# Attention with top-32, an MLP and routed experts on one core: top-k over folded scores, mask on ScalarE and GpSimd, exponential and turn moved back

## The chip, the cores and the metric

One core of a Trainium2 chip runs the whole program. The metric is the device time of one execution in microseconds (us); less is better. The engines are PE (TensorE; PEld its weight loads), DVE (VectorE), ACT (ScalarE), POOL (GpSimd) and SP (SyncE, which issues the loads).

## The reference, cut to what matters

Four batches of eight heads, 576 tokens, 64 wide:

```python
scores = scale * np.matmul(q, k.transpose(0, 1, 3, 2))          # 576 x 576 for each head
kth = np.partition(scores, -32, axis=-1)[..., -32:-31]
scores = np.where(scores >= kth, scores, -1000000000.0)
attn = np.exp(scores - np.max(scores, axis=-1, keepdims=True))
attn = attn / (np.sum(attn, axis=-1, keepdims=True) + 1e-09)
x = np.matmul(attn, v)                                         # then 2304 x 512
h = x @ w_in                                                   # 512 x 2048
g = np.where(h > 0.0, h, np.exp(np.minimum(h, 0.0)) - 1.0)
x = g @ w_out                                                  # 2048 x 512
# then one of eight experts (512 x 1024 x 512) for each token, by cosine similarity with expert_emb
```

## The kernel before, in words

**Tiles and slots.** A pair of heads takes nine tiles of 128 queries by 576 keys: four groups of two tiles (one for each head), and a fifth group with one mixed tile that holds the last 64 queries of both heads. There are 16 pairs, so 144 tiles. All engines run a loop over slots `s`, written out in Python, one tile entering in each; what an engine does in slot `s`, and in which order, is the order of the calls in its loop. Waits are on semaphores, and each engine works in order.

**One tile through the engines (before).** PE makes the scores in halves of 288 keys (`score`, L479 and L486) in two PSUM banks, ACT copies them to SBUF (`score_evac`, L682). DVE finds the 32 largest of each row: `eight` (L844) is a MAX8 over 576 columns, `without` (L848) a MATCH_REPLACE over 576 columns that strikes those eight out; four of the one and three of the other for a tile, the second half of one tile's chain interleaved with the first half of the next one's. `bias` (L853) gives the row maximum to ACT, which takes the exponential at once (`expo`, L688). DVE's `mask` (L859) compares the scores with the 32nd largest, multiplies the exponential with that and sums the row. PE turns the masked tile (`turn`, L494, five transposes; with the last tile of a group a sixth one, L498, turns the reciprocals that POOL spread out in `widen`, L355), two slots after the tile entered. ACT copies the turned tile (`turned`, L698), PE multiplies it with the values (`weigh`, L515), DVE multiplies with the reciprocals (`normalise`, L884).

**The MLP beside it.** `mlp_schedule` gives 71 positions for a batch, two to a slot: 32 chunks of the hidden layer (L534, 12 matmuls in fp32r: high and low parts), 32 sums of the second layer (L543, eight instructions each, some split finer so that there are 36 positions), and the row tiles (L552, L559), which go to DRAM. The MLP of batch `b` runs in the slots of batch `b + 1`, beginning `LAG` = 6 slots into it; so it starts in slot 42. For batches 0 to 2 it is beside attention; that of batch 3 is alone. A hidden chunk goes PE, ACT (L728 `Relu(-x)` to `elu_e`, L729 `Relu(x)` to `g`, which frees the PSUM bank, L732 `Exp`), POOL (L396, L398: minus one, add). Only in batch 3 DVE does POOL's part in one instruction (L933).

**After that** come the routing (DVE, PE) and a loop over the experts' tiles on PE (L643, L653).

The order of PE's loop in a slot: `prep` (turning the next pair's q and k, in slots 3 to 5 of a pair), `score(G, 0)` or nothing, `mlp` position 0, `turn(s - 2)`, `score(G, 1)`, `mlp` position 1, `weigh`. On DVE a wait in a chain is this:

```python
def settled(self, but=0):
    if self.n > but:
        dve.wait_ge(dve_step, self.n - but)
```

Of the kernel before, what the change touches and what calls it, by code (L numbers as in the profile page):

```python
# [5 lines left out]
ALU = mybir.AluOpType  # L6
# [7 lines left out]
P = 128  # L14
TOP_K = 32
NEG = -3.0e38


def attention_moe_program(nc, q, k, v, w_in, w_out, emb, tau, w1, w2, out):
# [26 lines left out]
    LAG = 6  # L46
# [5 lines left out]
    with ctx:  # L52
# [9 lines left out]
        ones = sbuf(ctx, "ones", [R, R])  # L62
# [3 lines left out]
        top = sbuf(ctx, "top", [P, 2, TOP_K])  # L66
        negmax = sbuf(ctx, "negmax", [P, 2])
        rowsum = sbuf(ctx, "rowsum", [P, 2, 2])
        rowrec = sbuf(ctx, "rowrec", [P, 2, 2])
        rec_b = sbuf(ctx, "rec_b", [P, 2, P])  # L70
# [17 lines left out]
        q_t = sbuf(first, "q_t", [P, 2, FULL * P])  # L88
# [4 lines left out]
        work = sbuf(first, "work", [P, 2, S])  # L93
        probs_t = sbuf(first, "probs_t", [P, 3, (NCH + 1) * P])
        x_f = sbuf(first, "x_f", [P, S])
        probs = sbuf(first, "probs", [P, 2, NCH * P])
        x2_t = sbuf(first, "x2_t", [P, KD, HS])
        elu_e = sbuf(first, "elu_e", [P, HS])
# [33 lines left out]
        def bank(name):  # L132
# [15 lines left out]
        rowmax, exp_done, mask_done, rec_done = (  # L148
            sem("rowmax"), sem("exp_done"), sem("mask_done"), sem("rec_done"))
        rec_wide = sem("rec_wide")  # L150
# [4 lines left out]
        elu_neg, elu_exp, elu_less = sem("elu_neg"), sem("elu_exp"), sem("elu_less")  # L155
# [53 lines left out]

        def x_at(t, b, pair, tok, n, parts=slice(0, P)):  # L210
            at = (NPAIR * b + pair) % RING * S + tok
            return t[parts, at:at + n]
# [3 lines left out]
        XT = 3  # L216
# [5 lines left out]
        def mlp_schedule():  # L222
# [13 lines left out]
            used, numbered = [0, 0], []  # L236
            for ops in positions:
                numbered.append([])
                for kind, blk, i, part, parts in ops:
                    bank_ = 0 if kind == "rows" else i % 2  # L240
                    if kind == "rows":

                        numbered[-1].append((kind, blk, i, used[1], 0, used[0]))
                        used[0] += 1
                        continue
                    numbered[-1].append((kind, blk, i, part, parts, used[bank_]))
                    if part == parts - 1:
                        used[bank_] += 1
            return numbered, used

        MLP_POSITIONS, BANK_USES = mlp_schedule()
# [8 lines left out]
        EARLY_SUMS = [op[5] + 1 for ops in MLP_POSITIONS for op in ops if op[0] == "rows"][RB - 1]  # L260
# [13 lines left out]
        def _(sp):  # L274
# [30 lines left out]
            sp.dma_start(work[0:E, 0, 0:DM], emb).then_inc(emb_in, 16)  # L305
# [36 lines left out]
        def _(pool):  # L342
# [7 lines left out]

            def widen(G):

                wait(pool, rec_done, G + 1)
                if G % GP < FULL:
                    pool.tensor_copy(rec_b[:, G % 2, :].rearrange("p (a d) -> p a d", a=2),  # L355
                                     rowrec[:, G % 2, :].unsqueeze(2).to_broadcast([P, 2, D])).then_inc(rec_wide, 1)
                else:
                    pool.tensor_copy(rec_b[:, G % 2, :], rowrec[:, G % 2, 0:1].to_broadcast([P, P])).then_inc(rec_wide, 1)
# [30 lines left out]
            def elu(mb, m, pos):  # L389
                for kind, blk, i, *_ in mlp_at(m, pos):  # L390
                    if kind == "hidden":
                        chunk = FC * 2 * mb + (FC * blk + i)
                        e, r = elu_e[:, :], g[:, i * HS:(i + 1) * HS]
                        wait(pool, elu_exp, chunk + 1)

                        pool.tensor_scalar(e, e, -1.0, 1.0, ALU.add, ALU.mult).then_inc(elu_less, 1)  # L396
                        wait(pool, elu_less, chunk + 1)
                        pool.tensor_tensor(r, r, e, ALU.add).then_inc(g_done, 1)  # L398

            for s in range(END):  # L400
                if 0 <= s - 2 < NT and ends_group(s - 2):
                    widen(group_of(s - 2))
# [5 lines left out]
                if step := mlp_slot(s):  # L408
# [690 lines left out]
```

## Time and profile before

| | |
|---|---|
| median of 3 runs | 1391.56 us (1389.16 to 1392.81) |
| the profiled execution | 1388.3 us, its span 1386.6 us |
| busy: PE, DVE, ACT, POOL | 1213.3, 932.9, 543.0, 247.0 us |
| slots 0 to 41, attention alone | 21.15 to 265.76 us |
| slots 42 to 143, attention and MLP of batches 0 to 2 | 265.76 to 883.5 us |
| the rest of batch 2's MLP | to 910.4 us |
| MLP of batch 3, routing, experts | to 1386.6 us |

A window's busy time is the union of an engine's instructions. Matmuls overlap: an instruction's duration is longer than the distance to the next one, and it is that distance which counts for a sum. The same holds for DVE and ACT where the next instruction need not wait.

### The profile page before, as it was taken

Reading aid. Unit: us, or ns where it says so; the run is one execution under the profiler, and the core shown is the slowest. Engines: PE = TensorE matmul, PEld = TensorE weight load, DVE = VectorE, ACT = ScalarE, POOL = GpSimd, SP = SyncE. Lnnn points to the kernel's source line nnn. Section 1 sums busy time; section 2 is a strip of 40 time slices with the busy share of each in tenths; the row PEclk is TensorE's granted clock in tenths of the full one; section 3 lists DMA queues with packets and bytes.
Section 4 is the critical chain, followed back from the end, with each engine's and each line's share of the span. In section 5 each row is a group of like instructions: output and inputs, shape, how many; then the busy total and the mean of one; then the engine's idle time right before and its main releaser. Section 6 shows DMA issues by size and latency. Waiting matters only on the chain.

```text
span 1386.6 us, 21604 instructions
## 1 busy us (share of the span) xinstructions
PE 1213.3 (88%) x7809; PEld 937.1 (68%) x7810; DVE 932.9 (67%) x2320; ACT 543.0 (39%) x1243; POOL 247.0 (18%) x391
## 2 busy tenths in 40 slices
PE   3656666799999999999999999999984999999996
PEld 2444444586787786687777677797864777677773
DVE  4999999999999999999999999610226110011100
ACT  3433443574474565465466456251620000000000
POOL 0212111140151042033023024000000111111111
PEclk9866666799999999999999999999996999999998
DMA  3141100100100100001011000000160354415100
GB/s 112 37 142 48 26 17 10 27 10 18 32 21 18 44 10 18 23 22 27 9 36 26 10 13 7 1 18 0 48 230 16 119 188 157 150 64 214 69 32 21
DMA packets 80121, 72.48 MB, mean 52 GB/s; under 512 B 60310, under 2 KB 60310, under 8 KB 79520
## 3 DMA queue, kind: packets, MB, share of 16 engines
q1 hardware_dynamic: 73584, 56.13, 12.9%
q0 software_dynamic: 3760, 10.49, 2.3%
q10 hardware_dynamic: 2688, 4.72, 1.2%
q8 instruction: 50, 0.82, 0.2%
q14 instruction: 39, 0.32, 0.1%
HBM read 61.88 MB, written 11.27 MB: 53 GB/s over the span
## 4 chain that ended last, share of the span: by engine, by line
PE 52%; DVE 36%; issue 5%; ACT 3%; POOL 2%; DMA 0%; SPq 0%; DVEq 0%; ACTq 0%; POOLq 0%
DVE work L848 15%; DVE top L844 14%; PE mlp L543 12%; PE sc L643 11%; PE pv_ps L653 10%; PE mlp L534 8%; DVE probs L859 5%; PE pv_ps L515 3%; PE sc L486 3%; PE tp L494 1%; POOL g L398 1%; PE mlp L552 1%; PE tp L623 1%; PE prep_ps L559 1%; POOL elu_e L396 1%
## 5 line engine op out<-in xcount | busy, mean ns | idle before, releaser
L844 DVE MAX8 top<-work 128x8 f32<-128x576 f32 x432 | 310.1, 744 | 0.1
L543 PE MATMUL mlp<-g,wout 128*128 128x288 f32 x1024 | 270.0, 411 | 0.0
L543 PEld LDWEIGHTS mlp<-g,wout 128*128 128x128 f32 x1024 | 187.7, 190 | 61.9 <-issue 17.4
L848 DVE MATCH_REPLACE8 work<-top,work 128x576 f32<-128x576 f32 x288 | 213.0, 740 | 0.0
L698 ACT COPY probs_t<-tp 128x640 f32<-128x640 f32 (+1 forms) x144 | 108.3, 752 | 191.2 <-PE tp L498 151.7
L494 PE MATMUL tp<-ident,probs 128*128 128x128 f32 x720 | 117.5, 300 | 59.0 <-DVE probs L859 59.0
L534 PE MATMUL mlp<-x_h,win_h 128*128 128x288 f32 x512 | 162.5, 317 | 0.1
L643 PEld LDWEIGHTS sc<-xg_t,w_exp 128*128 128x128 f32 x1344 | 154.6, 193 | 11.3 <-issue 11.3
L643 PE MATMUL sc<-xg_t,w_exp 128*128 x1344 | 154.9, 276 | 1.3 <-ACT act_tick L807 1.3
L534 PE MATMUL mlp<-x_h,win_l 128*128 128x288 f32 x512 | 151.5, 296 | 0.0
L534 PE MATMUL mlp<-x_l,win_h 128*128 128x288 f32 x512 | 151.5, 296 | 0.0
L494 PEld LDWEIGHTS tp<-ident,probs 128*128 128x128 f32 x720 | 93.7, 154 | 84.1 <-DVE probs L859 69.0
L682 ACT COPY scores<-sc 128x288 f32<-128x288 f32 x288 | 103.7, 407 | 114.6 <-PE sc L486 68.2
L653 PE MATMUL pv_ps<-w_exp,h_t 128*128 128x512 f32 x336 | 147.7, 592 | 0.0
L515 PE MATMUL pv_ps<-probs_t,vals 128*64 128x128 f32 (+1 forms) x1600 | 119.3, 307 | 15.4 <-DVE x_f L884 11.6
L515 PEld LDWEIGHTS pv_ps<-probs_t,vals 128*64 128x64 f32 x1600 | 99.3, 162 | 47.5 <-issue 34.5
L859 DVE SCALAR_TENSOR_TENSOR probs<-scores,top,probs 128x576 f32<-128x576 f32 x144 | 123.9, 861 | 0.5
L844 DVE MAX8 top<-scores 128x8 f32<-128x576 f32 x144 | 108.5, 754 | 20.6 <-ACT scores L682 20.3
L486 PE MATMUL sc<-k_t,q_t 64*128 64x288 f32 x512 | 114.7, 517 | 3.9 <-ACT scores L682 3.1
L688 ACT ACTIVATE probs<-scores,negmax 128x576 f32<-128x576 f32 x144 | 114.1, 792 | 0.0
L1067 DVE TENSOR_SCALAR y_all<-pv_ps,slots 128x512 f32 x21 | 15.8, 751 | 142.2 <-PE pv_ps L653 142.2
L653 PEld LDWEIGHTS pv_ps<-w_exp,h_t 128*128 128x128 f32 x336 | 62.2, 190 | 70.3 <-issue 70.3
(159 smaller groups left out, 1400.5 us busy)
## 6 DMA issues: line engine op xcount, KB each, us to landing
w_exp<-in_moe_w SPq DMA_DIRECT2D x16, 2048.0 KB, 13.7
x_rows<-g ACTq DMA_DIRECT2D x24, 192.0 KB, 2.1
raw_qk<-in_q SPq DMA_DIRECT2D x32, 128.0 KB, 2.4
raw_qk<-in_k SPq DMA_DIRECT2D x32, 128.0 KB, 2.4
vals<-in_v SPq DMA_DIRECT2D x32, 128.0 KB, 2.3
g<-in_moe_w_in SPq DMA_DIRECT2D x4, 1024.0 KB, 5.3
wout<-in_moe_w_out SPq DMA_DIRECT2D x1, 4096.0 KB, 15.9
raw_qk<-in_q SPq DMA_DIRECT2D x32, 16.0 KB, 2.2
```

Of the source, the lines that this page charges most:

```text
L486: pe.matmul(sc[n % 2][:, 0:HS], q_t[of, p % 2, g_ * P:(g_ + 1) * P], k_t[of, p % 2, keys], start=True, stop=True).then_inc(sc_half, 1)
L494: last = pe.transpose(tp[:, c * P:(c + 1) * P], probs[:, T % 2, c * P:(c + 1) * P], ident[:, :])
L515: mm = pe.matmul(pv_ps[of, 0:n], vals[:, p % 2, c, of], probs_t[:, buf, at:at + n], start=(c == 0), stop=(c == NCH - 1))
L534: mm = pe.matmul(mlp_ps[bank_][:, 0:HS], wp[:, c, i * P:(i + 1) * P], x_at(xp, mb, c, blk * HS, HS), start=(k_ == 1), stop=(k_ == 3 * KD))
L543: mm = pe.matmul(mlp_ps[bank_][:, 0:HS], wout[:, c, i * P:(i + 1) * P], g[:, c * HS:(c + 1) * HS], start=(c == 0), stop=(c == FC - 1))
L643: mm = pe.matmul(sc[half][:, fi * P:(fi + 1) * P], w_exp[:, par, c * F + f * P:c * F + (f + 1) * P], xg_t[:, bass.ds((s % 2) * (KD * P) + ...
L653: mm = pe.matmul(pv_ps[:, 0:DM], h_t[:, f, :], w_exp[:, par, KD * F + f * DM:KD * F + (f + 1) * DM], start=(f == 0), stop=(f == EC - 1))
L688: act.activation(probs[:, T % 2, 0:S], scores[:, T % NSC, :], ACT.Exp, bias=negmax[:, T % 2:T % 2 + 1], scale=SCALE).then_inc(exp_done, 1)
L698: act.copy(probs_t[:, T % 3, 0:n], tp[:, 0:n]).then_inc(pt_evac, 1)
L844: chain.mark(dve.max(top[:, T % 2, 8 * r:8 * r + 8], src))
L848: chain.mark(dve.match_replace(out=w_, in_to_replace=top[:, T % 2, 8 * r:8 * r + 8], in_values=scores[:, T % NSC, :] if r == 0 else w_, im ...
L859: dve.scalar_tensor_tensor(out=pr, in0=scores[:, T % NSC, :], scalar=top[:, T % 2, TOP_K - 1:TOP_K], in1=pr, op0=ALU.is_ge, op1=ALU.mult, ...
```

## The change

1. **Folded top-k.** A row of 576 scores is folded: `larger` (DVE) takes the maximum of key `i` and key `i + 288` (the second half straight from PSUM); POOL makes the other one of each pair as integers, `both_halves` (sum of the bit patterns) and `smaller` (sum minus larger). The 32 largest are found from the 32 largest of the larger ones (4 MAX8, 3 MATCH_REPLACE, 288 wide) and the 16 largest of the smaller ones (2 MAX8, 1 MATCH_REPLACE, 288 wide); `meet` and `threshold` (reductions over 17 pairs and 17 numbers) give the 32nd, `scaled` multiplies it with 2^100.
2. **Mask.** DVE's `mask` is gone. ACT's `drop` makes `Relu(BIG * (threshold - score))`, which is zero for what stays and huge otherwise; POOL's `mask` subtracts it from the scores; ACT's `expo` takes the exponential of that and sums the row with the same instruction; POOL's `total` adds 1e-9.
3. **Order.** `drop` in slot `s + 2` of tile `s`, `expo` in `s + 3`, `turn` in `s + 4` (before: exponential in `s`, turn in `s + 2`), the scores are made one slot earlier, both halves before the turn; `LAG` is 8. The reciprocals are turned on their own (`turn_rec`) into a free part of `pv_ps`, one slot later, copied by `turned_rec`, and `normalise` comes two slots later. `prep` moved to slots 5 and 6 of a pair, its third part to the end of slot 6; `q_t` has one buffer.
4. **ELU.** ACT does two instructions for a hidden chunk (`Relu(-x)`, `Exp`, in place in `g`), DVE one (`max(e - 1, x)`, reading `x` from PSUM), in all batches. POOL's two are gone. PSUM is freed by DVE's instruction.

```diff
-    LAG = 6
+    LAG = 8
@@ POOL
+            def total(G):
+                wait(pool, exp_done, last_of(G) + 1)
+                pool.tensor_scalar(sums_, sums_, 1e-9, 1.0, ALU.add, ALU.mult).then_inc(sum_done, 1)
+            def both_halves(T):
+                wait(pool, sc_evac, scores_of(T))
+                wait(pool, thr_done, T - 2)
+                pool.tensor_tensor(smaller_of[:, T % 3, :].bitcast(I32), s_[:, 0:HS], s_[:, HS:S], ALU.add).then_inc(summed_up, 1)
+            def smaller(T):
+                wait(pool, summed_up, T + 1)
+                wait(pool, larger_done, T + 1)
+                pool.tensor_tensor(m_, m_, larger_of[:, T % 4, :].bitcast(I32), ALU.subtract).then_inc(folded, 1)
-            def elu(mb, m, pos):
...
+            def mask(T):
+                wait(pool, dropped, T + 1)
+                pool.tensor_tensor(pr, scores[:, T % NSC, :], pr, ALU.subtract).then_inc(mask_done, 1)
@@ PE
             def turn(T):
-                wait(pe, mask_done, T + 1)
+                wait(pe, exp_done, T + 1)
-                if ends_group(T):
-                    wait(pe, rec_wide, G + 1)
-                    last = pe.transpose(tp[:, NCH * P:(NCH + 1) * P], rec_b[:, G % 2, :], ident[:, :])
+            def turn_rec(G):
+                wait(pe, rec_wide, G + 1)
+                pe.transpose(pv_ps[:, P:2 * P], rec_b[:, :], ident[:, :]).then_inc(rec_turned, 1)
...
-                        wait(pe, mlp_free[bank_], BANK_USES[bank_] * mb + n)
+                        wait(pe, mlp_free[bank_], ACT_USES[bank_] * mb + by_act)
+                        wait(pe, g_done, FC * 2 * mb + chunk if chunk else 0)
...
+                if 0 <= s - 5 < NT and ends_group(s - 5):
+                    turn_rec(group_of(s - 5))
+                if t in (5, 6) and p + 1 < NP:
+                    prep(p + 1, t - 5)
...
+                if G is not None:
+                    score(G, 1)
+                back = s - 4
...
+                if t == 6 and p + 1 < NP:
+                    prep(p + 1, 2)
@@ ACT
+            def drop(T):
+                wait(act, thr_done, T + 1)
+                wait(act, tr_done, T - 2)
+                act.activation(probs[:, T % 3, 0:S], scores[:, T % NSC, :], ACT.Relu,
+                               bias=thr[:, T % 2, 1:2], scale=-BIG).then_inc(dropped, 1)
             def expo(T):
+                wait(act, mask_done, T + 1)
+                wait(act, rec_done, G - 1)
...
+                               accum_out=rowsum[:, G % 2, head_of(T):head_of(T) + 1]).then_inc(exp_done, 1)
@@ DVE
+            def larger(T):
+                wait(dve, sc_evac, n + 1)
+                dve.tensor_tensor(larger_of[:, T % 4, :], scores[:, T % NSC, 0:HS], sc[n % 2][:, 0:HS],
+                                  ALU.max).then_inc(larger_done, 1)
-            def mask(T):
...
-                        dve.scalar_tensor_tensor(out=r, in0=e, scalar=-1.0, in1=r,
-                                                 op0=ALU.add, op1=ALU.add).then_inc(g_done, 1)
+                        dve.scalar_tensor_tensor(out=at, in0=at, scalar=-1.0, in1=mlp_ps[i % 2][:, 0:HS],
+                                                 op0=ALU.add, op1=ALU.max).then_inc(g_done, 1)
```

DVE in one slot without MLP, before (a slot that ends no group):

```order
L844 MAX top<-scores 128x8 [waits sc_evac]
L844 MAX top<-work 128x8 [waits dve_step]
L853 TENSOR_SCALAR negmax<-top 128x1 [waits dve_step]
L848 MATCH_REPLACE work<-top,scores 128x576
L848 MATCH_REPLACE work<-top,work 128x576 [waits dve_step]
L844 MAX top<-work 128x8 [waits dve_step] x2
L848 MATCH_REPLACE work<-top,work 128x576 [waits dve_step]
L884 TENSOR_TENSOR x_f<-pv_ps,probs_t 128x128 [waits pv_done]
L859 SCALAR_TENSOR_TENSOR probs,rowsum<-scores,top,probs 128x576 [waits exp_done,dve_step]
```

The same engine, one slot after the change, with no `larger` in it:

```order
L930 MAX top<-larger_of 128x8 [waits larger_done]
L935 MATCH_REPLACE larger_of<-top,larger_of 128x288 [waits dve_step]
L967 RECIPROCAL rowrec<-rowsum 128x2 [waits sum_done]
L930 MAX top<-larger_of 128x8 [waits dve_step]
L935 MATCH_REPLACE larger_of<-top,larger_of 128x288 [waits dve_step,folded]
L935 MATCH_REPLACE larger_of<-top,larger_of 128x288 [waits dve_step]
L930 MAX top<-smaller_of 128x8
L930 MAX top<-larger_of 128x8 [waits dve_step] x2
L949 TENSOR_REDUCE top<-top 128x17 [waits dve_step]
L942 TENSOR_SCALAR negmax<-top 128x1 [waits exp_done,dve_step]
L935 MATCH_REPLACE smaller_of<-top,smaller_of 128x288 [waits dve_step]
```

Behind it stand L955 (`threshold`), one more MAX8, L960 (`scaled`) and, in some slots, L979 (`normalise`) and the MLP's instruction. Seven wide instructions and the mask became ten of half the width and four narrow ones; a slot before a group's start has one or two `larger` (L926) too.

ACT in the hidden layer's slots, before:

```order
L728 ACTIVATE elu_e<-mlp 128x288 [waits mlp_done0,g_done]
L729 ACTIVATE g<-mlp 128x288
L732 ACTIVATE elu_e<-elu_e 128x288 [waits elu_neg]
L698 COPY probs_t<-tp 128x768 [waits pv_done,xn_done,tr_done]
L682 COPY scores<-sc 128x288 [waits sc_half] x2
L688 ACTIVATE probs<-scores,negmax 128x576 [waits tr_done,rowmax]
```

And ACT in such slots after the change:

```order
L744 ACTIVATE probs,rowsum<-probs,negmax 128x576 [waits rec_done,mask_done]
L759 COPY rec_t<-pv_ps 128x128 [waits xn_done,rec_turned]
L736 ACTIVATE probs<-scores,thr 128x576 [waits tr_done,thr_done]
L729 COPY scores<-sc 128x288 [waits sc_half,mask_done] x2
L786 ACTIVATE g<-mlp 128x288 [waits mlp_done0,x2_out]
L788 ACTIVATE g<-g 128x288 [waits elu_neg]
L729 COPY scores<-sc 128x288 [waits sc_half] x2
L753 COPY probs_t<-tp 128x640 [waits pv_done,tr_done]
```

The exponential (now L744) and `drop` (L736) stand ahead of the copies of the scores (now L729), and both halves of the scores are copied ahead of the turned tile (L753).

## Rows read from the trace of the kernel before

**Rows 1.** Busy time by stage; columns: stretch, busy of each engine, PEclk, DMA share, GB/s
```profile
21.15:265.76 244.61, 157.34 (x880) 105.33 (x880) 244.19 (x608) 99.90 (x197) 38.87 (x42) 0.71 0.16 45
265.76:883.50 617.74, 586.58 (x4222) 466.69 (x4221) 605.09 (x1507) 353.41 (x834) 156.29 (x259) 0.99 0.08 19
883.50:910.40 26.90, 24.85 (x157) 19.81 (x155) 4.42 (x15) 7.50 (x19) 1.98 (x3) 0.94 0.05 16
910.40:1031.80 121.40, 118.82 (x676) 104.32 (x676) 23.20 (x74) 44.48 (x122) 0.45 (x2) 0.98 0.21 77
```

**Rows 2.** Timeline, DVE in one slot: start us, duration us, engine, instruction
```profile
171.92 0.75 DVE L844 MAX8 top<-scores 128x8 f32<-128x576 f32 x1
172.59 0.74 DVE L844 MAX8 top<-work 128x8 f32<-128x576 f32 x1
...
173.30 0.08 DVE L848 MATCH_VALUE_LOAD work<-top,scores 128x8 f32 x1
...
174.03 0.08 DVE L848 MATCH_VALUE_LOAD work<-top,work 128x8 f32 x1
...
176.80 0.28 DVE L884 TENSOR_TENSOR x_f<-pv_ps,probs_t 128x128 f32<-128x128 f32 x1
177.00 0.81 DVE L859 SCALAR_TENSOR_TENSOR probs<-scores,top,probs 128x576 f32<-128x576 f32 x1
```

**Rows 3.** Groups by line, DVE: busy us, mean ns, idle before
```profile
L960 DVE TENSOR_TENSOR past<-small,edge 96x624 f32<-96x624 f32 x1 | 0.8, 803 | 0.0
...
L1040 DVE TENSOR_TENSOR lane_of<-lane,small 96x1024 f32<-96x1024 f32 x3 | 3.5, 1217 | 0.0
```

**Rows 4.** Groups by line, the MLP's instruction on DVE
```profile
L933 DVE SCALAR_TENSOR_TENSOR g<-probs,g 128x288 f32<-128x288 f32 x32 | 14.7, 459 | 91.6 <-ACT probs L732 91.6
```

**Rows 5.** Groups by line, POOL
```profile
L398 POOL TENSOR_TENSOR g<-g,elu_e 128x288 f32<-128x288 f32 x96 | 82.1, 855 | 8.0
...
L348 POOL TENSOR_TENSOR x_l<-x_f,x_h 128x576 fp32r<-128x576 f32 x16 | 22.5, 1409 | 11.9 <-ACT x_h L708 11.9
```

**Rows 6.** Timeline, a POOL instruction beside DVE's mask
```profile
500.75 1.46 POOL L398 TENSOR_TENSOR g<-g,elu_e 128x288 f32<-128x288 f32 x1
```

**Rows 7.** Timeline, PE in slots with MLP
```profile
404.56 0.76 PE L486 MATMUL sc<-k_t,q_t 64*128 64x288 f32 x4
405.25 0.40 PE L534 MATMUL mlp<-x_h,win_h 128*128 128x288 f32 x1
...
406.96 0.71 PE L494 MATMUL tp<-ident,probs 128*128 128x128 f32 x5
407.42 0.38 PE L534 MATMUL mlp<-x_h,win_h 128*128 128x288 f32 x1
...
450.77 2.11 PE L543 MATMUL mlp<-g,wout 128*128 128x288 f32 x8
452.80 1.31 PE L515 MATMUL pv_ps<-probs_t,vals 128*64 128x128 f32 x20
454.05 2.21 PE L543 MATMUL mlp<-g,wout 128*128 128x288 f32 x8
...
474.08 0.64 PE L552 MATMUL mlp<-ident,x_t 128*96 128x128 f32 x4
...
475.18 0.74 PE L494 MATMUL tp<-ident,probs 128*128 128x128 f32 x5
```

**Rows 8.** Waits, 265.76 to 910.4: engine line <- releaser: us, times, longest
```profile
PE tp L498 <- POOL rec_b L355: 22.9, 27, 1.6
```

**Rows 9.** Timeline, the first scores after the third part of prep
```profile
17.54 0.51 PEld L486 LDWEIGHTS sc<-k_t,q_t 64*128 64x128 f32 x4 [1.14 <-ACT k_t L671]
```

**Rows 10.** Groups by line, ACT
```profile
L688 ACT ACTIVATE probs<-scores,negmax 128x576 f32<-128x576 f32 x144 | 114.1, 792 | 0.0
...
L682 ACT COPY scores<-sc 128x288 f32<-128x288 f32 x288 | 103.7, 407 | 114.6 <-PE sc L486 68.2 <-PE sc L479 33.1 <-DVE probs L859 11.2
...
L732 ACT ACTIVATE elu_e<-elu_e 128x288 f32<-128x288 f32 x96 | 42.8, 446 | 0.0
```

More of the change, by code:

```diff
@@ L387, in _ @@
                                base=0, pattern=[[1, R]], channel_multiplier=-1).then_inc(consts, 1)
[L389 to L402 removed]
+            def mask(T):
+                pr = probs[:, T % 3, 0:S]
+                wait(pool, dropped, T + 1)
+                pool.tensor_tensor(pr, scores[:, T % NSC, :], pr, ALU.subtract).then_inc(mask_done, 1)
+            both_halves(0)
+            smaller(0)
+            for s in range(END):
+                if 0 <= s - 4 < NT and ends_group(s - 4):
+                    total(group_of(s - 4))
+                if s + 1 < NT:
+                    both_halves(s + 1)
+                    smaller(s + 1)
+                if 0 <= s - 2 < NT:
+                    mask(s - 2)
+                if 0 <= s - 4 < NT and ends_group(s - 4):
+                    widen(group_of(s - 4))
                 p, t = divmod(s - PT_ - XT, PT_)
@@ L547, in mlp @@
                     else:
[L550 removed]
+                        wait(pe, mlp_free[1], ACT_USES[1] * mb + part)
                         for c in range(KD):
@@ new lines, in without @@
+            def without(T, half, r):
+                w_ = folds(T, half)
+                chain.until(("eight", T, half, r))
+                chain.mark(dve.match_replace(out=w_, in_to_replace=ranks(T, half, 8 * r, 8 * r + 8), in_values=w_,
+                                             imm_value=NEG), ("without", T, half, r))
+            def bias(T):
+                chain.until(("eight", T, 0, 0))
+                wait(dve, exp_done, T - 2)
+                chain.mark(dve.tensor_scalar(negmax[:, T % 3:T % 3 + 1], top[:, T % 2, 0:1], -SCALE, None, ALU.mult),
+                           ("bias", T))
@@ L898, in slot @@
-                if summed is not None:
-                    total(summed)
+                    wait(dve, larger_done, new + 1)
+                    eight(new, 0, 0)
                 if old is not None:
-                    chain.settled(1 if new is not None else 0)
-                    eight(old, 2)
+                    without(old, 0, 1)
+                if s + 1 < NT and starts_group(s + 1):
+                    larger(s + 1)
                 if summed is not None:
                     reciprocal(summed)
+                if old is not None:
+                    chain.until(("without", old, 0, 1))
+                    eight(old, 0, 2)
@@ L905, in slot @@
                 if new is not None:
-                    chain.settled(1 if old is not None else 0)
-                    bias(new)
-                    without(new, 0)
+                    wait(dve, folded, new + 1)
+                    without(new, 0, 0)
                 if old is not None:
-                    chain.settled(1 if new is not None else 0)
-                    without(old, 2)
+                    without(old, 0, 2)
+                if s + 1 < NT and starts_group(s + 1) and not mixed(s + 1):
+                    larger(s + 2)
@@ L920, in slot @@
-                    without(new, 1)
+                    chain.until(("without", new, 0, 0))
+                    eight(new, 0, 1)
+                if old is not None:
+                    meet(old)
+                    bias(old)
+                if new is not None:
+                    without(new, 1, 0)
+                if old is not None:
+                    threshold(old)
+                if new is not None:
+                    chain.until(("without", new, 1, 0))
+                    eight(new, 1, 1)
```

252 lines of the change are left out of this document (137 added, 115 removed).

## The prediction

> **What bounds the kernel now.** I read the busy time by stage first [rows 1]. In slots 0 to 41 DVE is busy 244.19 of 244.61 us and PE 157 at a mean granted clock of 0.71: DVE is the bound, at 244.61 / 42 = 5.82 us a slot. In slots 42 to 143 (617.74 us, 6.06 a slot) DVE is busy 605 and PE 587 at 0.99: both are close to full. After 883.5 us DVE hardly matters, and after 910.4 the change touches only the ELU of the last batch. So there are two sums to make: A, the slots of DVE alone, and B, the stretch from the first MLP matmul to the last of batch 2 (617.74 + 26.90 = 644.6 us), in which PE takes over once DVE is shorter.
>
> **A: a DVE slot.** The timeline [rows 2] shows MAX8 instructions 172.59 - 171.92 = 0.67 us apart (duration 0.75) and MATCH_REPLACE, its value load included, 174.03 - 173.30 = 0.73 apart. Two wide DVE instructions of the routing give the slope: (1217 - 803) / (1024 - 624) = 1.035 ns a column [rows 3], so 288 columns less are 0.30 us less. A MAX8 over 288 is then 0.37 apart, a MATCH_REPLACE 0.43. The new slot:
> - 6 x 0.37 = 2.22 and 4 x 0.43 = 1.72;
> - one `larger` a tile: 0.459 long [rows 4], less the 0.07 by which neighbours overlap in [rows 2]: 0.39;
> - four narrow ones at about 0.06 to 0.09 apart (what the row maximum's scaling takes between 172.59 + 0.67 and 173.30, some 0.05, is their nearest measure): 0.27;
> - `normalise` 177.00 - 176.80 = 0.20 and the reciprocal 0.06, for five groups in nine slots: 0.14;
> - stalls where an instruction needs the one just before it, 0.08 to 0.11 each, about one a slot: 0.10.
>
> Together 4.84, say 4.85. Bounds: 4.75 with no stall; 5.8 if all ten pay their full length and not the distance (0.45 for the MAX8, 0.51 with the value load), since more of them hang on a near predecessor. I take the low end because the interleaved order leaves another instruction between most pairs.
>
> Against this speaks the Trainium skill, "VectorE: DVE Perf Modes", section on the TRN2 errata: a fixed latency is paid per instruction, so tiles should have 512 elements or more. With the fixed term of some 150 cycles that it gives, a 288-wide instruction is an estimated 0.46 us and ten of them with value loads about 5.0 us, a slot of 5.9, no gain in A. The row shows 0.67 for 576 columns where that page's estimate is 0.76, so the rows lean to the overlap.
>
> The other engines in A. POOL gets two 288-wide instructions (0.855 each, the nearest row being a float one) and one of 576 (1.409) [rows 5], with spreading about 3.4 us a slot, under 4.85. The same instruction took 1.46 while DVE's mask, with two operands in SBUF, ran [rows 6]; that mask is gone, and in the slots no DVE instruction has two SBUF inputs, so I take the undisturbed value. ACT gets `drop` (0.79) and loses nothing in A: two of 0.79, two halves at 0.41, one turned copy, some 3.2 us [rows 10]. Latency: `drop` waits for the end of DVE's slot, POOL's mask ends about 2.5 to 3.5 us later, the exponential follows in the next slot and PE turns in the one after; each hand-over has most of a slot to spare. The splitting of `w_in` (eight times) makes POOL slots too long early on: 5 us for that and the start. MLP now begins in slot 44: 21.15 + 44 x 4.85 + 5 = 239.6 us instead of 265.8. **A gains 26.2 us**; from +35 (4.75, no extra) to -16 (5.8).
>
> **B: PE's stretch.** I add up distances, not durations [rows 7]. A pair of score instructions 0.69, a hidden chunk 406.96 - 405.25 = 1.71, five transposes 0.46 to 0.55, a part of the second layer 2.03, weighing 1.25, a row tile 1.10. A pair of heads: scores 6.6, transposes 4.5 (nine), reciprocals 0.6, weighing 5.7, prep 1.2: 18.6, or 2.07 a slot. A batch of MLP: 32 x 1.71 + 32 x 2.03 + 6 x 1.10 = 126.3. Before: 102 x 2.07 + 3 x 126.3 = 590 of 644.6, so 55 us are idle. After: 100 slots of attention, 586. DVE would need 4.84 + 32/36 x 0.39 = 5.2 a slot, 520, so PE leads.
>
> What idles after:
> - gone: 22.9 us in which the sixth transpose waited for POOL's spread reciprocals [rows 8], which now has a whole slot;
> - smaller: the other 32, mostly PE kept back by DVE's pace; I keep 18 (8 to 32);
> - new: the third part of `prep` stands right ahead of the scores that need it. At the start this wait was 1.14 us [rows 9]; 11 pairs x 1.1 = 12;
> - new: the second half's scores wait for ACT's copies of the first, which stand behind the exponential, the reciprocals' copy and `drop` after the last hidden chunk (0.45 + 0.79 + 0.79 and a copy, [rows 10]); about 0.45 us where no weighing lies between, some 16 times: 7.
>
> Sum 37; 586 + 37 = 623. **B gains 21.6**; from +48 (only 10 idle) to +4 (idle stays 55). Two slots more of lag cost nothing by themselves: PE's work stays the same.
>
> **The last batch.** A bank is freed after `Relu`, `Exp` and DVE's instruction (0.41 + 0.45 + 0.46 and hand-overs, about 1.65 us [rows 4, 10]) and no longer after the two `Relu`; the other bank's chunk takes 1.58 there. Some 0.04 x 32: **minus 1.5**. Routing and experts, 355 us, stay.
>
> Sum: 26.2 + 21.6 - 1.5 = 46.3. The profiled execution took 1388.3 us and would take 1342; the median of the runs lies 3.3 above it, so 1391.6 - 46 = **1346 us**.
>
> **The rivals.**
> 1. PE packs better than I think: none of the new waits lasts, and DVE's slot is 4.75. A +35, B +42: 1391.6 - 75 = about 1317. For it: each new wait hangs on ACT, busy only 57% in B [rows 1]. Against: ACT's order. 0.13.
> 2. Short instructions do not overlap, or POOL and ACT hold DVE up now and then, a slot of 5.5: MLP starts at 268, A -2, B still about +21: 1372. The skill's rule above works this way. 0.12.
> 3. No change: DVE's slot stays near 5.8 and PE's idle time only changes its name. 0.04.
> 4. Slower: the hidden chunks. Their PSUM bank is freed by DVE at a late place in its slot, after ACT, whose queue holds about 5.5 us in a slot with scores and two chunks (0.79 + 0.79 + 4 x 0.35 + 0.6 + 4 x 0.43, rounded up with the reciprocals' copy). If PE's chunk and ACT's queue come one after the other instead of side by side, such a slot takes 5.5 + 1.71 = 7.2 instead of about 5.9. There are 48 hidden slots: 48 x 1.3 = 62, so 1346 + 62 = 1408. It decides the sign from 6.9 us a hidden slot on (46 / 48 = 0.96 more than forecast). For it: four engines in one ring, all in order. Against: two banks, and one slot of slack in every hand-over. 0.09. The Trainium skill, "GPSIMD Engine Reference", section 4.1, says that two-input elementwise work does not belong on GpSimd, about twice as slow as VectorE. The rows agree (0.855 against 0.459), and it would matter only if the integer form took over 2.0 us instead of 0.855, which would fill POOL's slot; I count it under this case.
>
> **How the numbers follow.** The forecast has 0.62, its own range 1325 to 1366. For 8 in 10 I reach to 1316 and to 1378, which takes in rival 1 and most of rival 2 and leaves out 3 and 4. A measurement of this kernel tells 0.3% (4 us) from no change. Faster: 0.62 + 0.13 + 0.12 = 0.87; the same 0.04; slower 0.09.
>
> **What would show it.** Slots without MLP about 4.85 us apart (first MAX8 to first MAX8 of the next tile), MAX8 over 288 0.37 apart; the first MLP matmul near 240 us; batch 3's first near 863; 36 slots of MLP near 210 us instead of 219; PE waiting for the third part of prep once a pair; no PE wait for spread reciprocals. Wrong would be: DVE idle for `folded` or for scores in the first stretch, POOL instructions much longer than 0.86 and 1.41, or hidden slots beyond 6.9 us.

## The result, and the profile after

The changed kernel takes 1473.97 us (median of 4 runs, 1469.21 to 1476.45), the kernel before on the same chip 1390.36 (1388.8 to 1392.81). The ratio is 1.0596, 95% interval 1.0562 to 1.063: slower by 84 us, where 46 us of gain were forecast. The profiled execution has a span of 1474.7 us.

The page of the kernel after, its busy time, clock, chain and the groups that answer to [rows 3 to 5]:

```profile
PE 1279.0 (87%) x7809; PEld 973.2 (66%) x7810; DVE 819.3 (56%) x3201; ACT 639.3 (43%) x1483; POOL 563.7 (38%) x711
...
PE 55%; issue 11%; POOL 8%; ACT 4%; DVE 1%; DMA 0%; DVEq 0%; POOLq 0%; ACTq 0%
...
L428 POOL TENSOR_TENSOR probs<-scores,probs 128x576 f32<-128x576 f32 x144 | 203.1, 1410 | 335.0 <-ACT probs L736 335.0
...
L930 DVE MAX8 top<-larger_of 128x8 f32<-128x288 f32 x576 | 245.9, 448 | 1.5
...
L935 DVE MATCH_REPLACE8 larger_of<-top,larger_of 128x288 f32<-128x288 f32 x432 | 189.2, 443 | 0.0
...
L729 ACT COPY scores<-sc 128x288 f32<-128x288 f32 x288 | 107.6, 396 | 132.3 <-POOL probs L428 93.1
...
L386 POOL TENSOR_TENSOR smaller_of<-scores 128x288 int32<-128x288 int32 x144 | 115.1, 799 | 81.2 <-ACT scores L729 72.8
```

Every instruction costs what the sum said or less: MAX8 0.448 us long, POOL's integer ones 0.80 (0.855 taken), its mask 1.41. DVE's whole busy time fell from 932.9 to 819.3 us. And DVE, which held 36% of the chain of the kernel before, is in 1% of it now; POOL, waits for issue and ACT stand there instead. So no instruction is too long: DVE is kept waiting.

Busy time by stage (stretch, then us and busy PE, PEld, DVE, ACT, POOL, clock, DMA share, GB/s), against [rows 1]:

```profile
21.00:302.90 281.90, 185.72 (x894) 120.22 (x893) 216.46 (x894) 137.06 (x309) 172.63 (x198) 0.66 0.14 40
302.90:955.00 652.10, 609.03 (x4157) 476.33 (x4158) 522.36 (x2108) 414.64 (x985) 335.69 (x418) 0.97 0.08 19
```

The first MLP matmul comes at 302.9 us (before 265.8), batch 3's first at 989.5 (before 910.4). Stretch A is 37 us longer than before, B 42 (686.6 against 644.6), the rest 9 (485.2 against 476.2). In A, DVE is busy 216 of 282 us, where it had next to no idle time before (244.19 of 244.61).

The waits between 21 and 989.5 us (engine, line <- whom: us in all, times, longest):

```profile
ACT scores L729 <- POOL probs L428: 93.1, 62, 5.0
PE sc L524 <- ACT scores L729: 77.6, 76, 4.1
ACT rec_t L759 <- PE pv_ps L538: 65.7, 46, 2.8
DVE rowrec L967 <- POOL rowsum L368: 49.4, 30, 4.7
DVE larger_of L926 <- ACT scores L729: 42.6, 30, 8.8
```

The first row is a wait that the prediction never names. Line 727 in `score_evac` lets ScalarE copy new scores only when `mask_done` has reached `T - NSC + 1`: with `NSC = 5` buffers, tile T goes where tile T - 5 was, and POOL's mask is the last to read that. Where a group of two tiles begins at s + 2, the scores of tiles s + 2 and s + 3 are now made in slot s, and the mask of tile s - 2 too. Tile s + 3 needs the buffer of tile s - 2: the copy waits for a mask of its own slot. That is so in 63 of the 144 slots, and the list has 62 such waits; a slot that makes no scores, or those of the mixed tile alone, has no such wait. A timeline of one slot and the next (start us, us, engine, instruction, idle before and whom it waited for):

```profile
76.27 0.29 POOL L375 COPY rec_b<-rowrec 128x128 f32<-128x128 f32 x1
76.71 0.14 DVE L960 TENSOR_SCALAR thr<-thr 128x1 f32<-128x1 f32 x1
...
80.02 0.78 ACT L744 ACTIVATE probs<-probs,negmax 128x576 f32<-128x576 f32 x1
...
80.18 2.40 PE L554 MATMUL pv_ps<-probs_t,vals 128*64 128x128 f32 x20 [0.78 <-ACT probs_t L753]
...
81.65 0.14 DVE L960 TENSOR_SCALAR thr<-thr 128x1 f32<-128x1 f32 x1
82.51 0.48 PE L538 MATMUL pv_ps<-ident,rec_b 128*128 128x128 f32 x1
...
83.02 0.27 ACT L759 COPY rec_t<-pv_ps 128x128 f32<-128x128 f32 x1 [2.13 <-PE pv_ps L538]
83.19 0.78 ACT L736 ACTIVATE probs<-scores,thr 128x576 f32<-128x576 f32 x1
...
84.04 1.40 POOL L428 TENSOR_TENSOR probs<-scores,probs 128x576 f32<-128x576 f32 x1 [5.11 <-ACT probs L736]
...
85.47 0.78 ACT L744 ACTIVATE probs<-probs,negmax 128x576 f32<-128x576 f32 x1 [0.69 <-POOL probs L428]
...
85.75 0.17 DVE L967 RECIPROCAL rowrec<-rowsum 128x2 f32<-128x2 f32 x1 [1.28 <-POOL rowsum L368]
...
86.25 0.76 ACT L736 ACTIVATE probs<-scores,thr 128x576 f32<-128x576 f32 x1
...
87.42 1.40 POOL L428 TENSOR_TENSOR probs<-scores,probs 128x576 f32<-128x576 f32 x1
...
88.86 0.70 ACT L729 COPY scores<-sc 128x288 f32<-128x288 f32 x2 [1.56 <-POOL probs L428]
...
89.31 1.32 PE L524 MATMUL sc<-k_t,q_t 64*128 64x288 f32 x2 [0.98 <-ACT scores L729]
```

Two things are to be seen. First the ring: `drop` 86.25, mask 87.42, copy 88.86, PE's scores 89.31, and behind them the second copy, DVE's `larger` and POOL's fold, which the next tile's threshold needs. Second, what stands ahead of `drop` on ScalarE. The tile of the `drop` at 83.19 had its threshold since 76.71 + 0.14 = 76.85 (the threshold of 81.65 is the next tile's, whose `drop` is that of 86.25). ScalarE stood at the copy of the turned reciprocals, which waited 2.13 us for PE until 83.02, and only then came `drop`. The mask of that tile was therefore late, the exponential waited for it until 85.47, and the next `drop` stood behind that exponential.

So `drop` does not wait for DVE here: one wait of 4.4 us is all that the trace has of it. Counted tile by tile in the trace, a `drop` begins 5.7 us on average after the end of its threshold in A (tiles 8 to 39) and 5.5 us in B (tiles 48 to 139).

### The profile page after: what moved, and what is told of

It reads as the page before. It is cut to its first block, busy times and chain, and to the rows that moved or that the text cites. A ratio compares the mean times of both kernels' runs of the same rounds, so it can differ in the third digit from the quotient of the medians.

```text
span 1474.7 us, 24124 instructions
## 1 busy us (share of the span) xinstructions
PE 1279.0 (87%) x7809; PEld 973.2 (66%) x7810; DVE 819.3 (56%) x3201; ACT 639.3 (43%) x1483; POOL 563.7 (38%) x711
## 4 chain that ended last, share of the span: by engine, by line
PE 55%; issue 11%; POOL 8%; ACT 4%; DVE 1%; DMA 0%; DVEq 0%; POOLq 0%; ACTq 0%
PE mlp L583 12%; PE sc L688 10%; PE pv_ps L698 10%; PE mlp L574 9%; POOL probs L428 4%; PE sc L524 3%; PE pv_ps L554 3%; PE tp L532 3%; POOL smaller_of L393 2%; POOL smaller_of L386 2%; ACT scores L729 1%; ACT probs L736 1%; PE mlp L592 1%; PE pv_ps L538 1%; PE tp L668 1%
## 5 line engine op out<-in xcount | busy, mean ns | idle before, releaser
L428 POOL TENSOR_TENSOR probs<-scores,probs 128x576 f32<-128x576 f32 x144 | 203.1, 1410 | 335.0 <-ACT probs L736 335.0
L524 PE MATMUL sc<-k_t,q_t 64*128 64x288 f32 x512 | 169.6, 531 | 102.3 <-ACT scores L729 78.1
L930 DVE MAX8 top<-larger_of 128x8 f32<-128x288 f32 x576 | 245.9, 448 | 1.5
L935 DVE MATCH_REPLACE8 larger_of<-top,larger_of 128x288 f32<-128x288 f32 x432 | 189.2, 443 | 0.0
L524 PEld LDWEIGHTS sc<-k_t,q_t 64*128 64x128 f32 x512 | 68.4, 216 | 174.9 <-ACT scores L729 127.9
L729 ACT COPY scores<-sc 128x288 f32<-128x288 f32 x288 | 107.6, 396 | 132.3 <-POOL probs L428 93.1
L1042 DVE SCALAR_TENSOR_TENSOR g<-g,mlp 128x288 f32<-128x288 f32 x128 | 57.9, 453 | 161.6 <-ACT g L788 161.0
L386 POOL TENSOR_TENSOR smaller_of<-scores 128x288 int32<-128x288 int32 x144 | 115.1, 799 | 81.2 <-ACT scores L729 72.8
L930 DVE MAX8 top<-smaller_of 128x8 f32<-128x288 f32 x288 | 131.7, 457 | 0.0
L532 PE MATMUL tp<-ident,probs 128*128 128x128 f32 x720 | 126.9, 316 | 0.1
L532 PEld LDWEIGHTS tp<-ident,probs 128*128 128x128 f32 x720 | 98.4, 162 | 39.7 <-issue 33.2
L393 POOL TENSOR_TENSOR smaller_of<-smaller_of,larger_of 128x288 int32<-128x288 int32 x144 | 114.9, 798 | 23.6 <-DVE larger_of L926 15.2
## 6 DMA issues: line engine op xcount, KB each, us to landing
w_exp<-in_moe_w SPq DMA_DIRECT2D x16, 2048.0 KB, 13.6
```

The costliest lines, as they stand in the source:

```text
L386: pool.tensor_tensor(smaller_of[:, T % 3, :].bitcast(I32), s_[:, 0:HS], s_[:, HS:S], ALU.add).then_inc(summed_up, 1)
L393: pool.tensor_tensor(m_, m_, larger_of[:, T % 4, :].bitcast(I32), ALU.subtract).then_inc(folded, 1)
L428: pool.tensor_tensor(pr, scores[:, T % NSC, :], pr, ALU.subtract).then_inc(mask_done, 1)
L524: pe.matmul(sc[n % 2][:, 0:HS], q_t[of, g_ * P:(g_ + 1) * P], k_t[of, p % 2, keys], start=True, stop=True).then_inc(sc_half, 1)
L532: last = pe.transpose(tp[:, c * P:(c + 1) * P], probs[:, T % 3, c * P:(c + 1) * P], ident[:, :])
L930: chain.mark(dve.max(ranks(T, half, 8 * r, 8 * r + 8), folds(T, half)), ("eight", T, half, r))
```

## Experiments

Ratios are to the kernel before, measured on the same chip, with 4 to 10 runs of a version and 7 to 15 of the kernel before. The experiments ran on four chips, on which the kernel before took 1389.55 to 1390.36 us, so a difference between two versions carries up to 1 us from that. Theory 1 is the ring through the score buffers; theory 2 is the hidden chunks' way through DVE, or PE's clock; theory 3 is the order in POOL's queue, where the mask stands behind the fold; each expectation says what a rival would give. A sixth score buffer needs room in SBUF, so the first run is a control that only saves memory.

**1. The control, five buffers.** `smaller_of` has 2 buffers for 3, `q_diag` 1 for 2, `probs` no padding (the fifth transpose is 64 wide), with the waits that follow from it.

```
-        smaller_of = sbuf(first, "smaller_of", [P, 3, HS])
-        probs = sbuf(first, "probs", [P, 3, NCH * P])
+        smaller_of = sbuf(first, "smaller_of", [P, 2, HS])
+        probs = sbuf(first, "probs", [P, 3, S])
```

> Control for the next run: the changed kernel with the SBUF savings that a sixth score buffer needs (smaller_of in two buffers, q_diag in one, probs without the padding columns, whose transpose becomes 64 wide; scaled waits one instruction more), but still five score buffers. All theories expect 1474 us within 6, the copy of the scores (ACT) still waiting about 90 us in all for POOL's mask.

1475.54 us, ratio 1.0621 (1.0596 to 1.0645): the same as the changed kernel.

**2. Six score buffers.** One more edit on the control:

```
-    NSC = FULL + 1
+    NSC = FULL + 2
```

> As the control, with six score buffers instead of five, so the copy of tile s+3's scores in slot s no longer waits for the mask of tile s-2 made in the same slot, but for that of s-3. Theory 1 (the reused score buffer closes a ring drop, mask, copy, scores, copy, fold within one slot): ACT's wait for POOL's mask before a copy of scores falls from 93 us to under 15, slots without MLP fall from 6.4 to about 5.0 us, the first MLP matmul comes near 250 instead of 303 us, in all 1474 - 53 - 35 = about 1385 us. Theory 2 (the ELU's ring through DVE in the hidden slots, or PE's clock, makes it slow): within 15 us of the control. Theory 3 (POOL's order): some 30 us less, since the mask is still queued behind the fold.

1396.06 us, ratio 1.0042 (1.0028 to 1.0056). One number gives 79.5 us back, 32 before the first MLP matmul (it comes at 269.8 us, in run 1 at 302.0) and 41 between it and batch 3's first (642.8 against 683.5). Theory 2 falls with that, and theory 3, which gave it 30. The size that theory 1 named, 1385 us with the first MLP matmul near 250, was not reached. ScalarE's wait for POOL's mask is gone from the list of waits, and PE's for ScalarE falls from 77.6 us to 32; the stages are 248.8 and 642.8 us:

```profile
PE sc L523 <- ACT scores L729: 32.0, 31, 2.6
DVE rowrec L967 <- POOL rowsum L368: 36.9, 28, 4.6
...
21.00:269.80 248.80, 169.62 (x894) 115.70 (x893) 218.34 (x887) 136.11 (x309) 172.34 (x198) 0.69 0.16 45
269.80:912.60 642.80, 612.87 (x4363) 488.77 (x4363) 532.64 (x2122) 420.63 (x1013) 340.56 (x426) 0.98 0.08 19
```

**3 and 4. POOL's mask ahead of its fold**, with five buffers (3) and with six (4). In the ring the mask is queued behind POOL's two integer instructions; this takes them out from ahead of it.

```
+                if 0 <= s - 2 < NT:
+                    mask(s - 2)
                 if s + 1 < NT:
                     both_halves(s + 1)
                     smaller(s + 1)
-                if 0 <= s - 2 < NT:
-                    mask(s - 2)
```

> The changed kernel with one thing moved: POOL's mask of tile s-2 stands ahead of both_halves and smaller of tile s+1 in POOL's slot. Theory 1: the copy of the scores still waits for the mask (1.41 us) right behind drop, so the ring stays, only the long waits of up to 5 us go: about 1440 us. Theory 3 (the order on POOL is the cause): near 1385 us. Theory 2: no change, 1474.

> Six score buffers and POOL's mask first. Theory 1: no more than 10 us from the run with six score buffers alone. Theory 3: clearly below it, by 20 us or more.

Run 3, on the changed kernel itself: 1485.17 us, ratio 1.0675 (1.0651 to 1.0699). Run 4: 1410.24, ratio 1.0151 (1.0129 to 1.0173). They are 11 and 14 us worse than without the edit. A miss, for theory 3 and for what theory 1 expected too (1440 in run 3, at most 10 us in run 4). There was little to gain on POOL: without the edit the mask of the median tile starts 0.08 us after its `drop` ends (335 us of POOL's idle time are put down to `drop`). And the sums and the fold, which DVE needs, can now wait behind the mask: DVE's wait for the row sums grows from 49.4 to 100.2 us in run 3, that for the fold from 0.6 to 32.2.

**5 to 8. What is left, with six buffers.** Three reorderings, each alone. 5: DVE's `reciprocal` behind `scaled`, not ahead of the old tile's third `eight`, since there the threshold waits with it for POOL's sums. 6: the third part of `prep` on PE and ACT right behind the second half of the scores, not at the slot's end. 7, on ScalarE:

```
-                if 0 <= s - 3 < NT:
-                    expo(s - 3)
-                if 0 <= s - 5 < NT and ends_group(s - 5):
-                    turned_rec(group_of(s - 5))
                 if 0 <= s - 2 < NT:
                     drop(s - 2)
                 G = scored_in(s)
                 if G is not None:
                     score_evac(G, 0)
+                if 0 <= s - 3 < NT:
+                    expo(s - 3)
+                if 0 <= s - 5 < NT and ends_group(s - 5):
+                    turned_rec(group_of(s - 5))
```

> Six score buffers, and DVE's reciprocal moved from the fourth place of its slot to behind scaled. Theory R (early in its slot DVE waits for POOL's total, which stands behind the whole POOL slot, the splitting of w_in included): DVE's wait for the row sums falls from 37 us to under 8, slots without MLP from 5.65 to about 5.1, the first MLP matmul near 247 instead of 269.8 us, in all 1396 - 22 = about 1374. Rival (those waits only take the place of others, for the folded scores that the same POOL slot makes): within 6 us of 1396.

> Six score buffers, and prep's third part moved from the end of slot 6 of a pair to just behind the second half of the scores, on PE and ACT. Theory P (PE waits for ACT's three small copies once a pair): PE's 20.5 us of waiting for k_t go, some 12 of them beside the MLP count: about 1384. Rival (another wait of the ring takes their place): within 4 us of 1396.

> Six score buffers, and ACT's exponential and the copy of the reciprocals moved behind the copy of the first half of the scores. Theory C (PE's second half of the scores waits for those copies, 32 us): 10 to 20 us less, about 1381. Rival (the exponential then comes later to the turn and POOL's total, which cost more): 1396 to 1410.

> Six score buffers, late reciprocal and early prep together. If theories R and P both hold the gains add up: about 1362. If one bound hides the other, within 5 us of the better of the two.

| run | us | ratio (95%) | against run 2 |
|---|---|---|---|
| 5 late reciprocal | 1385.95 | 0.9974 (0.9961 to 0.9986) | -10.1 |
| 6 early third part | 1386.38 | 0.9978 (0.9966 to 0.9991) | -9.7 |
| 7 exponential behind copy | 1382.80 | 0.9951 (0.9933 to 0.9968) | -13.3 |
| 8 = 5 and 6 | 1377.35 | 0.9917 (0.99 to 0.9934) | -18.7 |

The reciprocal gave 10 us, not 22: its wait falls from 36.9 us to 6.9, but three other waits of DVE grow by 26 together (for the scores 32.6 to 44.4, before `normalise` 19.6 to 23.9, for the hidden chunks' exponential 106.5 to 116.6). Most of that wait only changes its place. Run 8 is 18.7 under run 2, where 5 and 6 add up to 19.8; the 1362 of its expectation rested on the 22.

**9 to 11. All three, and the last batch.** Run 9 has the three reorderings. Run 10 has run 2's order, but in the last batch the hidden chunks take turns in four PSUM banks:

```
+        def hidden_ps(mb, i):
+            return (sc if mb == B - 1 and i % 4 >= 2 else mlp_ps)[i % 2]
```

Run 11 has both.

> The six-score-buffer kernel with all three reorderings: DVE's reciprocal behind the scaled threshold, preparation's third part behind the second half of the scores, and on ScalarE the exponential and the turned reciprocals behind the copy of the first half of the scores. The two first added (8.7 and 9.7 apart, 18.7 together), so theory 'separate waits' expects the third's 13 us to come on top, since it shortens the copy of the first half that both others leave alone: 1377.3 - 13 = 1364, ratio to before 0.982. Rival: the third shortens the same wait for the scores as the early third part of the preparation did (both let PE's scores go sooner), so they overlap: 1370 to 1375, ratio 0.987 to 0.990.

> The six-score-buffer kernel; in the last batch alone, where attention is over, hidden chunks take turns in four PSUM banks (the two of the MLP and the two of the scores) in place of two. Theory: with the bank freed by DVE's last step and not by ScalarE's, a chunk in the last batch takes 1.66 to 1.72 us in place of 1.58, 32 chunks, so 3 to 4 us come back: 1392.5, ratio to the six-buffer kernel 0.9975, to before 1.002. Rival: the last batch is longer for another reason (clock, the first chunk's start), then nothing moves: 1396. The nearest look at it is the distance between the hidden chunks' last matmuls.

> The three reorderings and the four banks together. Gains of separate stages should add: whatever the kernel with three orders takes, less what the four banks gave (3 to 4 us). If 1364 and 3.5, then 1360.5, ratio to before 0.979.

Run 9: 1363.69 us, 0.9794 (0.9774 to 0.9814), as expected if the gains add. Run 10: 1395.38, 1.0039 (1.0025 to 1.0054), 0.7 us against run 2, so 3 to 4 were not found. Run 11: 1359.74, 0.9775 (0.976 to 0.9789), 4 us under run 9 by the medians, but the ranges overlap (1357.32 to 1363.63 against 1357.52 to 1364.86) and the spans are 1361.9 and 1362.0, so I count no gain. The distances in run 10 say where it went. In run 2 the chunks' first `Relu` come 1.58 and 1.80 us apart in turn, with four banks 1.58 each time, and the first 16 chunks take 24.2 us in place of 25.8. But among the next 16 stand row tiles, whose neighbours are 4.4 to 5.4 us apart, and there it lost 0.5.

Run 11 is the fastest version measured, 2.25% under the kernel before. Its first stretch is 227.1 us (before 244.6) and its second 629.7 (before 644.6):

```profile
21.00:248.10 227.10, 159.89 (x893) 106.55 (x893) 215.68 (x879) 135.82 (x310) 172.03 (x198) 0.77 0.18 49
248.10:877.80 629.70, 609.97 (x4364) 485.58 (x4364) 532.19 (x2130) 419.58 (x1014) 343.85 (x427) 0.98 0.08 20
```

**12. The best version with five buffers.** `NSC` of run 11 set back.

> The best kernel (three reorderings, four banks) with one number set back: five score buffers in place of six. Theory: the ring through the masked tile's buffer is the bound of the attention stretches whatever the order within a slot, so the loss returns. The reciprocal's and the third part's places still save what they saved elsewhere (some 18 us), but the exponential, now behind the copy that waits for the mask, is later too, so its 13 us turn into a loss: 1475 - 18 + 0 to 13 = 1457 to 1470, ratio to before 1.048 to 1.057. Rival: the four edits act on the same chain as the sixth buffer, and most of their gain comes with five too: 1475 - 36 = 1439, ratio 1.035. If it comes under 1400, the sixth buffer was not what the other orders needed.

1408.11 us, ratio 1.0137 (1.0116 to 1.0158). Both theories missed, and it is the run that taught most. I had the sign of the exponential's place wrong: behind the copy it stands no longer ahead of `drop`, where the ring begins. With the order as changed the sixth buffer is worth 79.5 us, with the better order 48. Turned round, the better order (with the four banks) is worth 36 us with six buffers and 67 with five. So the missing buffer is not the whole cause.

**13 to 15. Which order, with five buffers.** 13 is the control with run 7's edit; 14 moves `turned_rec` alone and leaves the exponential; 15 has the edits of runs 5 and 6.

> The slim kernel with five score buffers (1475.5); only ScalarE's exponential and the copy of the turned reciprocals moved behind its copy of the first half of the scores. Theory 5 (two hand-overs long): the ring drop, mask, copy, second half of the scores is late because drop itself is late, and on ScalarE the exponential (0.98 us) and the turned reciprocals (0.26 and a wait for TensorE, 65.7 us in 46 waits) stand ahead of drop; this gives 30 to 50 us: 1425 to 1445, ratio 1.025 to 1.04. Theory 6 (DVE's reciprocal): the one delay that matters is DVE's wait for the sums ahead of the threshold; then this gives what it gave with six buffers, 13 us: 1462.

> The same five-buffer kernel; only the copy of the turned reciprocals moved behind the copy of the first half of the scores, the exponential stays ahead of drop. Theory 5: some half of the former run's gain, 80 groups at 1.4 us of wait and 0.26 of copy, two thirds of it seen: 1450. Theory 6: nothing, 1475.

> The same five-buffer kernel with the two other orders: DVE's reciprocal behind the scaled threshold and the third part of the preparation behind the second half of the scores. Theory 5: 18.7 us as with six buffers, 1457, ratio 1.049. Theory 6: DVE's wait for the sums (49.4 us in 30 waits) holds the threshold, so drop, so the ring; this gives 40 us or more: 1435 or less, ratio under 1.033.

| run | us | ratio (95%) | against run 1 |
|---|---|---|---|
| 13 exponential and turned reciprocals | 1418.63 | 1.0212 (1.0195 to 1.0229) | -56.9 |
| 14 turned reciprocals alone | 1454.41 | 1.0452 (1.0428 to 1.0476) | -21.1 |
| 15 reciprocal and third part | 1472.73 | 1.0585 (1.0554 to 1.0616) | -2.8 |

Of theory 5 the cause holds: what stands ahead of `drop` on ScalarE counts, the turned reciprocals alone for 21 us, and the exponential for another 36 behind them. Its sizes were off: run 13 came under its 1425 to 1445, and run 15, where it expected 1457, gave next to nothing. Theory 6 falls. Of the waits of run 13, ScalarE's for the turned reciprocals is down from 65.2 us in run 1 to 39.7, and POOL's for `drop` from 327.2 to 173.9:

```profile
POOL probs L427 <- ACT probs L736: 173.9, 118, 5.1
...
ACT scores L729 <- POOL probs L427: 73.9, 58, 4.4
...
ACT rec_t L759 <- PE pv_ps L538: 39.7, 30, 2.8
```

The ring is still there (73.9 us of ScalarE waiting for the mask), but it starts earlier. From the end of a tile's threshold to its `drop`, on average over the tiles named above, it takes 5.4 us in A and 5.4 in B in run 1, 3.7 and 5.0 in run 14, 2.2 and 3.6 in run 13 (with six buffers, run 2, 3.1 and 4.7). Its timeline in one slot:

```profile
172.85 0.78 ACT L736 ACTIVATE probs<-scores,thr 128x576 f32<-128x576 f32 x1
...
173.71 1.40 POOL L427 TENSOR_TENSOR probs<-scores,probs 128x576 f32<-128x576 f32 x1 [1.00 <-ACT probs L736]
...
175.15 0.40 ACT L729 COPY scores<-sc 128x288 f32<-128x288 f32 x1 [1.23 <-POOL probs L427]
175.44 0.78 ACT L744 ACTIVATE probs<-probs,negmax 128x576 f32<-128x576 f32 x1
175.60 1.32 PE L523 MATMUL sc<-k_t,q_t 64*128 64x288 f32 x2 [0.87 <-ACT scores L729]
```

From `drop` to PE it takes 175.60 - 172.85 = 2.75 us (3.06 in the slot shown of the changed kernel), and the exponential (0.78 us, with 0.19 for the reading of its sum) now runs beside PE instead of ahead of the ring.

By stage the two cures differ. Run 13's first MLP matmul comes at 268.6 us: before it, the order gives 33 us with five buffers, as much as the sixth buffer gives with the old order (32). Between that matmul and batch 3's first it gives 22 (661.6 against 683.5), the sixth buffer 41. Run 14 gives 20 before the first MLP matmul and nothing behind it (687.1). And run 12, which is run 13 with the edits of 5 and 6 and the four banks, is 10.5 us under it: with ScalarE's order put right, what gave 2.8 us in run 15 gives more.

## Why the prediction was wrong

**The step that failed** is in part A: "`drop` waits for the end of DVE's slot, POOL's mask ends about 2.5 to 3.5 us later, the exponential follows in the next slot and PE turns in the one after; each hand-over has most of a slot to spare". It looks at the way forward alone, from the scores to the turn, and leaves out the way back: the mask also frees a buffer, and the copy that waits for it stands in the same slot. Hand-overs with a slot to spare were counted for each result that is used, and none for a buffer that comes free. Before, POOL had no part in this and the scores were made later; the change moves both ends towards each other and leaves `NSC` at five. With that one number right the kernel takes 1396, and the error falls from 128 us to 50. The first words of the sentence are wrong as well: `drop` began 5.7 us after its threshold in A and 5.5 in B, held by ScalarE's own queue.

**The second error** is the order on ScalarE. I added ScalarE's work (3.2 us in a slot of 4.85) and took that for room. The sum is right, 136.11 us busy in the 44 slots of run 2's first stretch, 3.1 a slot, but the engine works in order: an exponential and a wait for TensorE of up to 2.8 us stood ahead of `drop`. Its price depends on the first error: 13 us with six buffers, 57 with five. Half of it was in the prediction: "the second half's scores wait for ACT's copies of the first, which stand behind the exponential, the reciprocals' copy and `drop`". I priced that at 7 us, in B. In its profile run 7 took 2.7 us out of B (640.1 against 642.8) and 13.4 out of A (first MLP matmul at 256.4 against 269.8), where I had set nothing for it.

Point by point:
- **DVE's instructions**: right. The distance of the MAX8 in the timeline of the kernel after is 180.10 - 179.73 = 0.37 us as forecast, and in run 9 a slot that nothing holds up is 4.55 us long without a `larger` and 5.3 with two, from the first MAX8 of one tile to that of the next: 4.90 on average, against 4.85.
- **The Trainium skill's rule** ("VectorE: DVE Perf Modes", the TRN2 errata, a fixed latency for each instruction), by which the prediction estimated 0.46 us an instruction. As a duration that is what the trace shows, 0.448 and 0.457 us. The distance, which is what the sum needs, is 0.37: the second MAX8 below starts at 180.10, before the first one ends (179.73 + 0.45). The row of 576 columns had hinted at it, 0.67 apart and 0.75 long where the estimate is 0.76.

```profile
179.73 0.45 DVE L930 MAX8 top<-smaller_of 128x8 f32<-128x288 f32 x1
180.10 0.80 DVE L930 MAX8 top<-larger_of 128x8 f32<-128x288 f32 x2
```

- **A, 26.2 us of gain**: minus 37. With six buffers it was minus 4, in run 11 plus 17.7 (first MLP matmul at 248.1, forecast 239.6). The 8.5 us left over are for the most part two slots in each nine, in run 9 of 5.5 to 6.3 and 6.1 to 6.7 us where 4.55 would do. Both end in a wait of DVE for the copy of the turned reciprocals, of 0.5 to 1.2 us in the first and 1.7 to 1.9 in the second. 5 us were set aside for the splitting of `w_in`.
- **B, a gain of 21.6**: minus 42. With six buffers plus 2, in run 11 plus 15 (629.7 us against 623). The new wait for the third part of `prep`, forecast at 12 us, was 9.7 by run 6 (13.6 of B in its profile, 629.2 against 642.8), a hit. The 22.9 us in which a transpose waited for POOL's spread reciprocals [rows 8] did go from PE. But their copy has a wait of its own on ScalarE now, the 65.7 us before `rec_t`, and that I had not followed. It is a wait for PE's order, at least in the slot shown: POOL had spread the reciprocals at 76.27, PE turned them at 82.51, right behind the weighing that began at 80.18.
- **The last batch, minus 1.5**: about minus 5 in run 2 (92.0 us from the first chunk's `Relu` to the last one's, before 87.3), and about minus 7 in run 9 and in the changed kernel (94.6 and 94.2). That the bank comes free only after DVE fits run 10, in which other banks bring the distance back to 1.58; the size was off: chunks 1.69 us apart on average where the forecast had 1.62, and a row tile's neighbours 4.4 us apart, where they had been 3.8.
- **Rival 4** named the right kind of cause, "four engines in one ring, all in order", and set it in the wrong ring, that of the hidden chunks, at 62 us and 9 in 100. Its sign came true all the same: the 54 slots in which hidden chunks pass ScalarE took 7.0 us on average, beyond the 6.9 it names; with the sixth score buffer, and the chunks' banks as they were, they took 6.4. Its argument against, "one slot of slack in every hand-over", is the failed step once more. The Trainium skill's rule beside it ("GPSIMD Engine Reference", section 4.1) was not the cause: the integer instructions took 0.80 us and the mask 1.41.

Open is whether the last 14 us to the forecast can be had: 486 us behind batch 3's first matmul in run 9 against 476 before is only in part explained by the banks, and I tried nothing on the two long slots in each nine.

## What to carry to other kernels

When stages are moved a slot apart, list for every ring of buffers the slot of the last reader of T - n and the slot of the writer of T; if they are the same, the ring is a chain through every engine between them, and one more buffer may be worth more than the whole change. Then look at what stands in the queue ahead of the first link: an instruction that nobody needs before the next slot, above all one with a wait of its own, belongs behind it. A sum of busy times per slot shows neither.

## What was not expected

- One buffer of scores: 79.5 us of 1475, though no engine was busy for more than 87% of the span. The wait that carries its name, 93.1 us in 62 cases, is only the tenth row of the whole list of waits, far below POOL's 335.0 for `drop`.
- The worth of an edit hangs on the other one: that on ScalarE gave 13.3 us with six buffers and 56.9 with five; the two others gave 18.7 with six and 2.8 with five.
- POOL's two-input integer instruction of 288 columns took 0.80 us, and so did the float one: the 0.855 of its row [rows 5] is a mean in which 87 of 96 took 0.80 and nine took 1.19 to 1.46. In each of these nine DVE's mask, which reads two operands from SBUF, had begun first and still ran. In 13 others POOL had begun first: it kept its 0.80, and there the mask took 0.91 to 1.34 us instead of 0.81. No instruction of this kind is left on DVE in the attention slots of the kernel after, and POOL's 144 additions there took 0.79 to 0.82.
